# Attention constants reordered, their waits moved on TensorE, and 52 matmuls of ones ahead of the first chunk

## The reference

```
attention: for each batch and head, over 768 steps
    y_t   = r_t . (state + u*k_t (x) v_t)
    state = w*state + k_t (x) v_t
mixture:   logits = x @ w_gate; the best of 8 experts takes the token (capacity 384)
    out = gate * (relu(x @ w1[e]) @ w2[e])
last:      out = relu(x @ w_in)^2 @ w_out
```

## Time and profile before

| | us |
|---|---|
| median of 3 runs | 436.42 |
| lowest, highest | 435.76, 439.98 |
| profiled execution | 438.97 |
| its span | 436.9 |

### The profile page before, as it was taken

How to read it: one execution, slowest core, us unless ns; L and a number is a source line. 1 busy time by engine, 2 the same in 40 slices (tenths; PEclk the granted TensorE clock), 3 DMA queues, 4 the chain that set the end, 5 groups by cost and what they waited for, 6 DMA issues and landing times.

```text
span 436.9 us, 10114 instructions
## 1 busy us (share of the span) xinstructions
PE 408.9 (94%) x3954; PEld 380.7 (87%) x3954; DVE 257.7 (59%) x442; ACT 211.5 (48%) x414; POOL 64.7 (15%) x75
## 2 busy tenths in 40 slices
PE   0889999499999999999999999999999999999994
PEld 0878898289999999999998889989988988998984
DVE  5375675777877667668657455356445537545331
ACT  2355668325655646646545444445354444444321
POOL 3653550162012022000000000004000004000003
PEclk9998999579999999999999999999999999999998
DMA  7976987069965566556463314224322323200002
GB/s 210 249 227 166 280 290 221 21 202 333 341 240 201 184 219 222 163 209 207 155 216 96 122 72 142 75 74 145 143 72 83 133 72 126 90 1 0 1 0 78
DMA packets 18736, 66.44 MB, mean 152 GB/s; under 512 B 2889, under 2 KB 7642, under 8 KB 18705
## 3 DMA queue, kind: packets, MB, share of 16 engines
q1 hardware_dynamic: 16912, 61.32, 43.4%
q0 software_dynamic: 1792, 4.72, 2.8%
HBM read 59.74 MB, written 7.08 MB: 153 GB/s over the span
## 4 chain that ended last, share of the span: by engine, by line
PE 75%; DVE 4%; issue 2%; ACT 1%; DVEq 0%; POOLq 0%; ACTq 0%
PE score_banks L569 18%; PE y_banks L569 17%; PE gate_bank L592 6%; PE spare_bank L592 6%; PE state_bank L592 6%; PE sum_bank L592 6%; PE gate_bank L582 5%; PE state_bank L582 5%; PE sum_bank L582 5%; PE spare_bank L609 1%; PE spare_bank L559 1%; DVE ylo L1104 0%; PE score_banks L550 0%; DVE hlo L1085 0%; ACT cv L758 0%
## 5 line engine op out<-in xcount | busy, mean ns | idle before, releaser
L914 DVE TENSOR_TENSOR wlo<-raw,whi 128x1536 fp32r<-128x1536 f32 x56 | 98.4, 1758 | 91.5 <-ACT whi L719 88.8
L719 ACT ACTIVATE whi<-raw 128x1536 fp32r<-128x1536 f32 x56 | 83.3, 1489 | 83.3 <-PE spare_bank L592 47.6
L1081 DVE TENSOR_TENSOR sq<-rl 128x512 f32<-128x512 f32 x48 | 32.9, 689 | 30.0 <-ACT rl L795 30.0
L447 POOL DMA_INDIRECT out<-osb,oidx x12 | 13.0, 1081 | 247.9 <-ACT osb L853 245.0
L418 POOL DMA_INDIRECT xg<-attention_out,gidx x16 | 19.5, 1217 | 90.2 <-PE spare_bank L559 64.1
L1085 DVE TENSOR_TENSOR hlo<-sq,hhi 128x512 fp32r<-128x512 f32 x48 | 30.9, 686 | 0.0
L569 PE MATMUL y_banks<-yhi,whi 128*128 (+1 forms) x72 | 28.4, 395 | 0.0
L569 PE MATMUL score_banks<-ylo,whi 128*128 (+1 forms) x72 | 28.4, 395 | 0.0
L569 PE MATMUL score_banks<-yhi,whi 128*128 (+1 forms) x72 | 28.4, 395 | 0.0
L569 PE MATMUL y_banks<-yhi,wlo 128*128 (+1 forms) x72 | 28.4, 395 | 0.0
L569 PE MATMUL score_banks<-yhi,wlo 128*128 (+1 forms) x72 | 28.4, 395 | 0.0
(11 more groups left out here) (217 smaller groups left out, 1139.4 us busy)
## 6 DMA issues: line engine op xcount, KB each, us to landing
raw<-in_wts SPq DMA_DIRECT2D x56, 768.0 KB, 4.3
tok<-in_tok SPq DMA_DIRECT2D x12, 416.0 KB, 5.1
feat<-in_feat SPq DMA_DIRECT2D x16, 192.0 KB, 3.5
vT<-in_vT SPq DMA_DIRECT2D x12, 192.0 KB, 4.4
attention_out<-x_sb SPq DMA_DIRECT2D x12, 192.0 KB, 3.8
out<-rl SPq DMA_DIRECT2D x12, 192.0 KB, 5.8
feat<-in_feat SPq DMA_DIRECT2D x4, 448.0 KB, 8.2
xg<-attention_out,gidx POOLq DMA_INDIRECT x16, 4.8
```

Of the source, the lines that this page charges most:

```text
L447: nc.gpsimd.indirect_dma_start(out=out[:, :], out_offset=bass.IndirectOffsetOnAxis(ap=oidx[:, t:t + 1], axis=0), in_=osb[:, t, :], in_offs ...
L719: return nc.scalar.activation(dst, src, ACT.Copy)
L914: v.tensor_tensor(wlo[:, r, :], raw[:, r, :], whi[:, r, :].bitcast(F32), ALU.subtract).then_inc(w_lo, 1)
L1081: v.tensor_tensor(sq[:, ft, :], rl[:, ft, :], rl[:, ft, :], ALU.mult).then_inc(h_sq, 1)
```

## The change

52 matmuls of `ones_b` by itself stand at the head of TensorE's list; GpSimd sets `ones_b` first for them, under its own semaphore. Tr is made by ScalarE, in four pieces, and TensorE waits for each piece. Its transposes go to `spare_bank`. VectorE makes `dec` and `uw` ahead of chunk 0's features, and does the small memsets before it waits for w. The wait for `decm` stands at the state matmuls, the wait for `tokw` is gone (VectorE has its own, ahead of `khat`), and GpSimd no longer waits for Tr.

```diff
@@ gpsimd
+            nc.gpsimd.memset(ones_b[:, :], 1.0).then_inc(ones_set, 1)
             nc.gpsimd.memset(ident[:, :], 0.0).then_inc(pool_step, 1)
...
-            nc.gpsimd.memset(ones_b[:, :], 1.0).then_inc(consts, 1)
...
-            pool.wait_ge(table_ready, 1)
             pool.wait_ge(prod_ready, 1)
@@ tensor
+            pe.wait_ge(ones_set, 1)
+            for _ in range(52):
+                pe.matmul(spare[:, 0:P], ones_b[:, :], ones_b[:, :], start=True, stop=True)
             pe.wait_ge(consts, 1)
-            pe.wait_ge(table_ready, 1)
             for g in range(G):
-                mm = pe.transpose(ps_x[:, g * ROWS:(g + 1) * ROWS], Tr[0:ROWS, g, :], ident[0:ROWS, 0:ROWS])
+                pe.wait_ge(table_ready, g + 1)
+                mm = pe.transpose(spare[:, g * ROWS:(g + 1) * ROWS], Tr[0:ROWS, g, :], ident[0:ROWS, 0:ROWS])
...
             pe.wait_ge(in_wg, 16)
-            pe.wait_ge(tokw_ready, 2)
             pe.wait_ge(uw_ready, 3)
-            pe.wait_ge(decm_ready, G)
...
                     pe.wait_ge(khat_ready, n + 1)
+                    pe.wait_ge(decm_ready, G)
                     pe.wait_ge(state_ready, n + 2)
@@ scalar
-            act.wait_ge(tokw_psum, 1)
-            for o in range(2):
-                copy(tokw[:, :].rearrange("p (g o d) -> p g o d", g=G, o=2)[:, :, o, :],
-                     ps_x[:, 0:G * ROWS].rearrange("p (g q) -> p g q", g=G)[:, :, ODD * o:ODD * o + D]).then_inc(tokw_ready, 1)
...
-            act.wait_ge(consts, 1)
             act.wait_ge(dec_ready, 1)
             for g in range(G):
+                nc.scalar.activation(Tr[0:ROWS, g, :], T[0:ROWS, g, 127::-1], ACT.Copy, scale=dec[0:ROWS, g:g + 1]).then_inc(table_ready, 1)
+            act.wait_ge(consts, 1)
+            for g in range(G):
                 nc.scalar.activation(decm[0:ROWS, g, :], ident[0:ROWS, :], ACT.Copy, scale=dec[0:ROWS, g:g + 1]).then_inc(decm_ready, 1)
+            act.wait_ge(tokw_psum, 1)
+            for o in range(2):
+                copy(tokw[:, :].rearrange("p (g o d) -> p g o d", g=G, o=2)[:, :, o, :],
+                     spare[:, 0:G * ROWS].rearrange("p (g q) -> p g q", g=G)[:, :, ODD * o:ODD * o + D]).then_inc(tokw_ready, 1)
@@ vector
             v.memset(T[w, :, 64:65], 1.0)
+            v.memset(uw[:, :, :], 0.0).then_inc(uw_ready, 1)
             v.memset(oh[:, :, :], 0.0)
+            for j, s in enumerate((vx_ready, csum_ready, heads_ready, heads_ready, masked, masked)):
+                v.memset(free[:, j:j + 1], 0.0).then_inc(s, 1)
...
             dve.wait_ge(in_w, 16)
...
+            v.tensor_tensor(dec[w, :], T[w, :, 128], T[w, :, 128], ALU.mult).then_inc(dec_ready, 1)
+            dve.wait_ge(in_u, 16)
+            dve.wait_ge(uw_ready, 1)
+            for o in range(2):
+                rows = slice(ODD * o, ODD * o + D)
+                v.tensor_tensor(uw[rows, :, o], ucol[rows, :], wcol[rows, :], ALU.mult).then_inc(uw_ready, 1)
             dve.wait_ge(in_feat[0], 16)
...
             v.tensor_tensor(prod[0][w, :], Rd[0][w, :], feat[0][w, 1, :], ALU.mult).then_inc(prod_ready, 1)
-            v.tensor_tensor(dec[w, :], T[w, :, 128], T[w, :, 128], ALU.mult).then_inc(dec_ready, 1)
-            dve.wait_ge(dec_ready, 1)
-            v.tensor_tensor(Tr[w, :, :], T[w, :, 127::-1], dec[w, :].unsqueeze(2).to_broadcast([ROWS, G, C]), ALU.mult).then_inc(table_ready, 1)
-            v.memset(uw[:, :, :], 0.0).then_inc(uw_ready, 1)
...
             dve.wait_ge(consts, CONSTS)
```

More of the change, by code:

```diff
@@ L57 @@
 PARTS = 5
-CONSTS = 10
+CONSTS = 9
 SLOTS = 4
@@ L177, in build @@
         consts = sem("consts")
+        ones_set = sem("ones_set")
         zeros_set = sem("zeros_set")
@@ L871, in _ @@
             v.memset(T[w, :, 64:65], 1.0)
+            v.memset(uw[:, :, :], 0.0).then_inc(uw_ready, 1)
             v.memset(oh[:, :, :], 0.0)
+            for j, s in enumerate((vx_ready, csum_ready, heads_ready, heads_ready, masked, masked)):
+                v.memset(free[:, j:j + 1], 0.0).then_inc(s, 1)
+            v.memset(gout[:, :], 0.0).then_inc(y_ready, 1)
+            v.memset(off[:, :], 0.0).then_inc(unit_done, 1)
+            v.memset(start[:, :], 0.0).then_inc(o_act, 1)
+            v.memset(kept[:, :], 0.0).then_inc(o_dve, 1)
             dve.wait_ge(in_w, 16)
```

## The result

The median of 20 runs is 434.78 us (432.73 to 438.90), against 437.78 (435.22 to 442.0) in 20 runs of the kernel before. The ratio is 0.9931 [0.9911, 0.9952]: 3.0 us gained, or 0.7%, where I forecast 430.0, with 428.5 to 432 for my own case and 425.5 to 433.8 in all. Ratios leave out the few executions that were far slower than the others of their kernel: three of the six of g_merge, one of h_slots2, and two of the kernel before in the jobs of the experiments. The profiled execution took 435.96 us with a span of 433.8, where before had 438.97 and 436.9.

What follows compares the result with a forecast made beforehand. TensorE's list was taken as the bound, delayed at its start. Chunk 4 7.6 us earlier, less 0.8 for clock spells, gave 6.8: 432.2 from the profiled 438.97, 429.6 at the median, taken as 430.0; range 425.5 to 433.8.

Steps and rivals of the forecast that it cites:

- my own case: Whole kernel: the main forecast, 430.0 us, from 428.5 to 432; chance 0.50.
- Part 1: Start: with Tr on ScalarE and fewer waits, TensorE starts chunk 0 at 7.6 us, 4.7 us earlier.
- Part 2: Ahead of chunk 0: 52 matmuls take 5.5 us and raise TensorE's clock; chunk 0 takes 4.7 us, not 8.15.
- first rival: Chunk 0 stays at the lower clock: 432.5 us, or 433.3 with a further spell; chance 0.17.
- Part 3: Chunk 1: its Rd on GpSimd, bound by landing features, lets it start at 13.1 us, 7.3 us earlier.
- Part 4: Chunks 0 to 3: waits for code at 5.2 us per block put chunk 4 at 30.8 us, 7.6 us earlier.
- given back: First chunks: code or features come 1 us later per block, losing 3 to 4 us; 433 to 434; chance 0.13.
- slower rival: Block 213's and later code packets queue behind the first loads; at 8.5 us per packet, 442 us; chance 0.05.
- Part 5: First chunks: one to two spells of low clock likely, some 0.6 us each, 0.8 us in all.
- second rival: First chunks: no waits for code, gain 10.9 us less 0.8, giving 425.9 to 426.5; chance 0.10.

Runs made afterwards that it cites:

- g_merge: Changed kernel with matmuls of gate values, scores, bonus sums and both parts of y taking 128 tokens at once, not two halves of 64; ratio 1.0238.
- h_slots2: Changed kernel with two chunks unrolled in place of four, so only chunks 0 and 1 are loaded at the start; ratio 0.9941.
- g_after: The changed kernel itself, unaltered, run again in another job; ratio to the kernel before 0.9951.
- f_dve1: Changed kernel with chunk 1's two decayed products made on VectorE in place of GpSimd; ratio to the kernel before 0.9919.
- g_light: Changed kernel with first tokens and gate values of chunks 1 to 3 zeroed, not loaded; ratio 1.19 means nothing, chunk 4 starts at 32.79 us.
- g_hold2: Changed kernel with the load of chunk n, from chunk 2, waiting for the scores of chunk n-2; ratio to the kernel before 0.9923.
- f_loop_dve1_hold: Changed kernel with the 52 matmuls looped 13 by 4, chunk 1's products on VectorE, loads of chunks 2 and 3 held until chunk 0's scores; ratio 0.9946.
- j_tokfirst: Changed kernel with two slots in place of four and each chunk's tokens sent for once their buffer is free; ratio 0.9845, median 431.37 us.
- e_ones_only: Kernel before with only the 52 matmuls of ones added and ones_b set first; ratio to the kernel before 0.9923.

## Why the prediction was wrong

**Part 1 held.** Its terms add up to 7.5 (5.4, 1.27 and 0.8), not 7.6. Chunk 0 was forecast at 7.6 and started at 8.11; Tr took 1.28 us on ScalarE against 1.27. In that execution Rd came late; the same kernel had chunk 0 at 7.66 in g_after.

**Part 2 held.** The 52 matmuls took 5.66 us (forecast 5.5), the clock was up from 6.5, the masked scores took 1.10. The first rival (0.17) did not occur.

**Part 3 was 0.9 us short.** Chunk 1 started at 13.97, not 13.1. GpSimd could start on chunk 1's features at 11.21, and the first product on GpSimd took 1.44 us, not 1.18. By f_dve1 this cost nothing.

**Part 4 failed, by the size of one term.** The stalls stand at pairs 213, 337 and 461, as counted. But I took 5.2 us from each block entry to the next, from two intervals of the kernel before, and applied it to another stretch. (The packet sent for at a block's entry is that of the next block, not of the next but one, as I had put it: each stall ended 2.3 to 3.1 us after it.) From the entry of the block at pair 89 (9.3 by its place in chunk 0) to 16.08 it took 6.8 us, then 7.7 and 5.65. Three blocks at 5.2 are 15.6 us; from 16.08 on, the two that TensorE had to wait for took 13.4, and there was no stall at 585. The start of chunk 4 was put at 30.8; it came at 34.91. The rows that would have warned me were the DMA share of 0.85 in the window that I measured in the earlier trace rows, and the landings of the first loads, up to 20.9 us, in the earlier trace rows: the requests moved from behind these loads into the midst of them, where the share was 1.02 to 1.06. g_light and g_hold2 show that the packet comes sooner when the loads leave room.

This is the rival that I called given back (0.13; 433 to 434; 434.78 came), and half of it is the slower rival's mechanism: that packets queue behind the first loads. Its price there was 7.1 us or more for each packet. In the changed kernel's profile only one block took that long (7.7), in g_after two (7.5 and 8.75), and at 585 the first had no wait any more and the second one of 0.50. My prices for that rival did not follow from its own condition either: a packet sent for at 8.7 that is there at 20.9 + 1.4 takes 13.6 us, not 7.1 or 8.5. My reason against it, a packet that crossed in about 1 us at 0.85, was about the crossing, which stayed at 0.9 to 1.4 us in both profiles. The time goes before it starts.

The Trainium skill (Runtime: NRT & Kernel Launch, Instruction fetch mechanics) has the costs of the block's boundary mostly hidden. The traces don't agree in the first pass: 0.20 to 4.81 us idle at about half of the boundaries.

**Part 5 was too small, and its sum was wrong in kind.** A spell of low clock was priced at 1.65 us, of which 0.6 was to be left, from the one of the kernel before (33.9 to 37.3, 3.4 us). It lasted 6.8 us, behind two idle spots of 1.16 and 1.17. That it overlaps with a wait for code was right: it hid nearly all of the second one, 0.64 left. So clock and code are not two terms that add but two bounds, of which the later decides (g_light, f_loop_dve1_hold). In the block at pair 213 both were late at once: at the low clock TensorE needed until 23.16 for it, and the code let it go on at 23.80.

**The sum and the range.** 6.8 us were forecast on the profiled execution and 3.0 came. Another 1.4 us of the miss are not of the mechanism: the median of three runs before, 436.42, was low, 20 runs gave 437.78, and I had counted the 430.0 from the three. That the lead at chunk 4 passes through to the end was right: in the kernels with four slots and no edit inside the loop, whose clock was up by chunk 4, it is 397.2 to 398.9 us from there. The second rival (no waits for code, 0.10) did not occur: no kernel with four slots was free of them, and j_tokfirst, with two, gains 6.4 of its 10.1. The range reached 433.8, since I put part of the given-back case outside it, though nothing in the trace showed the 5.2 to hold amid the loads.

## What to carry over

Where the first pass of an unrolled loop still has its code to fetch, price it by the loads that are in flight at the moment at which the boundary will fall, not at the moment at which it fell. Here a start made earlier moved those requests into the burst of first loads, and half of its gain ended there. Two slots in place of four, with the tokens sent for in the order of need, doubled what the earlier start alone gave; whether by less code or by fewer first loads is open.

## What was not expected of the hardware

- A packet of code of 16 KB takes 0.9 to 1.4 us to cross in the first 40 us of the kernel before, the changed one and g_light, but behind the block at pair 213 it starts 1.2 us after block entry at a DMA share up to 0.4 and 4.4 to 6.5 at 1.04 to 1.06.
- A loop of four chunks, 560 pairs or some 70 KB of code (16 KB for each 124 pairs), sends for code in its first round; in the changed kernel one packet is left after that of 31.14 until 74 us, at 54.41, and chunks 4 to 6 start 4.5 and 5.1 us apart.
- The same float32 work takes 6.5 us a chunk with 128-column weights, and 4.5 with two halves of 64 (g_merge beside h_slots2).
- In e_ones_only the clock fell within 2.56 us of idle, and with chunk 0's small matmuls under way from 12.02 it rose only at 18.6, where with the 52 matmuls of ones it rose in under 5.5 us (1.07 to 6.53).
